# Attention and an MLP mixer on one core: the products with v as quarters of the TensorE array

## The reference

```python
def _attn_ref(q, k, v):                      # each (4, 8, 576, 64)
    ...
    q_rot, k_rot = (rotate(q), rotate(k))
    scores = scale * np.matmul(q_rot, k_rot.transpose(0, 1, 3, 2))
    scores = scores - np.max(scores, axis=-1, keepdims=True)
    attn = np.exp(scores)
    attn = attn / (np.sum(attn, axis=-1, keepdims=True) + 1e-09)
    return np.matmul(attn, v)

def _moe_ref(x, w_tok1, w_tok2, w_ch1, w_ch2):   # x is (4, 576, 512)
    xt = x.transpose(0, 2, 1)
    h = np.maximum(xt @ w_tok1, 0.0) @ w_tok2
    u = x + h.transpose(0, 2, 1)
    h2 = np.maximum(u @ w_ch1, 0.0) @ w_ch2
    return u + h2
```

## Time and profile before

| | |
|---|---|
| median of two runs | 676.19 us (674.8 to 677.58) |
| profiled execution, its own time | 677.07 us |
| span of its records | 675.2 us |
| granted clock of TensorE, mean | 1.00 |
| busy: PE, PEld, DVE, ACT, POOL | 650.1, 627.6, 449.6, 390.2, 296.1 us |

### The profile page before, as it was taken

The page is one execution under the profiler, slowest core; times in us unless marked ns, Lnnn a source line. Parts: engine busy times, 40 slices in busy tenths (PEclk is TensorE's granted clock), DMA queues, the critical chain, the costliest instruction groups (busy, mean ns, idle before and its releaser), DMA issues.

```text
span 675.2 us, 19627 instructions
## 1 busy us (share of the span) xinstructions
PE 650.1 (96%) x7796; PEld 627.6 (93%) x7796; DVE 449.6 (67%) x844; ACT 390.2 (58%) x725; POOL 296.1 (44%) x276
## 2 busy tenths in 40 slices
PE   3999999999999999999999999999999999999997
PEld 2999999999999999999899999999999999999997
DVE  5576766666766666666545598548974489644895
ACT  3455556565555565665547355677646775476753
POOL 4656567766665566522570000484004840048300
PEclk9999999999999999999999999999999999999999
DMA  4234433344433544311600233100031000310002
GB/s 131 73 99 116 130 87 107 101 109 112 116 108 104 149 111 134 87 53 34 205 2 1 63 126 102 48 1 2 2 102 47 0 0 2 99 48 1 1 2 71
DMA packets 52177, 48.73 MB, mean 72 GB/s; under 512 B 15104, under 2 KB 44352, under 8 KB 52096
## 3 DMA queue, kind: packets, MB, share of 16 engines
q1 hardware_dynamic: 51792, 47.52, 24.8%
q10 hardware_dynamic: 304, 0.07, 0.0%
HBM read 30.77 MB, written 9.44 MB: 60 GB/s over the span
## 4 chain that ended last, share of the span: by engine, by line
PE 96%; ACT 1%; DVE 1%; issue 0%; DVEq 0%
PE rest L648 24%; PE slot L604 10%; PE slot L1158 8%; PE slot L1160 8%; PE slot L1159 8%; PE rest L543 7%; PE rest L1158 6%; PE rest L1160 6%; PE rest L1159 6%; PE slot L600 3%; PE slot L1190 2%; PE rest L1190 2%; PE slot L543 1%; PE rest L224 1%; PE rest L221 1%; ACT pt L762 1%
## 5 line engine op out<-in xcount | busy, mean ns | idle before, releaser
L648 PE MATMUL rest<-v,pt 64*128 64x65 f32 x2304 | 152.5, 272 | 7.8 <-ACT pt L762 7.1
L648 PEld LDWEIGHTS rest<-v,pt 64*128 64x128 f32 x2304 | 147.0, 189 | 10.9 <-ACT pt L762 9.4
L840 DVE TENSOR_REDUCE neg_max<-slot 128x1 f32<-128x576 f32 x144 | 108.6, 756 | 71.1 <-PE slot L604 67.8
L1149 POOL TENSOR_TENSOR w_ch_part<-w_ch_sums,w_ch_part 128x512 fp32r<-128x512 f32 x21 | 31.0, 1475 | 178.0 <-ACT w_ch_part L1400 178.0
L762 ACT ACTIVATE pt<-rest 128x320 f32<-128x320 f32 x128 | 55.6, 435 | 88.6 <-PE rest L543 88.6
L1464 ACT ACTIVATE pieces<-h 128x288 fp32r<-128x288 f32 x168 | 73.8, 444 | 49.9 <-PE slot L1160 26.4
L604 PE MATMUL slot<-turned_k,turned_q 64*128 64x288 f32 x256 | 88.2, 436 | 2.3 <-ACT moved_q L776 1.6
L604 PE MATMUL slot<-moved_k,moved_q 64*128 64x288 f32 x256 | 88.2, 436 | 0.0
L1555 DVE TENSOR_TENSOR pieces<-h,pieces 128x288 fp32r<-128x288 f32 x168 | 74.3, 452 | 9.3 <-ACT pieces L1464 8.8
L851 DVE COPY pt<-rest 128x320 f32<-128x320 f32 x128 | 61.7, 482 | 14.8 <-PE rest L543 14.8
L751 ACT ACTIVATE prob_a<-slot,neg_max 128x576 f32<-128x576 f32 x80 | 59.2, 740 | 15.9 <-DVE neg_max L840 12.8
(11 more groups left out here) (248 smaller groups left out, 1922.8 us busy)
## 6 DMA issues: line engine op xcount, KB each, us to landing
moved_q<-turned_q SPq DMA_DIRECT2D x31, 160.0 KB, 2.5
raw_qk<-in_q_dram SPq DMA_DIRECT2D x16, 256.0 KB, 2.6
raw_v<-in_v_dram SPq DMA_DIRECT2D x16, 256.0 KB, 2.7
x_scratch<-x_pair SPq DMA_DIRECT2D x16, 256.0 KB, 2.0
stage_or_x<-x_scratch SPq DMA_DIRECT2D x16, 256.0 KB, 4.0
raw_qk<-in_k_dram SPq DMA_DIRECT2D x15, 256.0 KB, 2.9
w_ch_whole<-in_moe_w_ch_dram SPq DMA_DIRECT2D x8, 384.0 KB, 3.5
w_ch_A_whole<-in_moe_w_ch_dram SPq DMA_DIRECT2D x4, 768.0 KB, 7.8
```

The source lines that it names most:

```text
L648: return pe.matmul(rest[:, 2 + r, at:at + V], x[rows, j, :], w[rows, j, :], start=begins, stop=ends, skip_group_check=True)
L840: dve.tensor_reduce(neg_max[p % 2][:, i:i + 1], score_slot(p, i)[:, :, 0:HALF], AX.XY, ALU.max, negate=True).then_inc(maxed, 1)
```

## The change

Each product with v is issued twice, once for 64 of the 128 queries and once for the other 64. The weights become 64 keys by 64 queries, and the output of a product goes to partitions 0 to 63 or to partitions 64 to 127 of the same bank: rows and columns of the array are both used in halves. The same 65 columns of v stream past both. Semaphores, the order of steps and all other instructions stay.

```diff
             def add(r, n, x, w, j, begins=False, ends=False):
                 rows = (top, low)[r]
                 at = (n - HEADS["AB"[n >= G]][0]) * V
-                return pe.matmul(rest[:, 2 + r, at:at + V], x[rows, j, :], w[rows, j, :], start=begins, stop=ends, skip_group_check=True)
+                for half in (top, low):
+                    mm = pe.matmul(rest[half, 2 + r, at:at + V], x[rows, j, half], w[rows, j, :], start=begins, stop=ends, skip_group_check=True)
+                return mm
```

## The result

The changed kernel takes **653.39 us** (median of 652.32 and 654.46) against 676.19 before: a ratio of 0.9653, 95% interval 0.9604 to 0.9702. It is faster by 23 us. The forecast was 640 us in 608 to 724. The profiled execution took 654.46 us, its span is 652.7, the clock of TensorE 1.00.

The account below looks back on a forecast made before the run. The prediction took PE, busy 96% of the span, to bound the kernel, and the load of 128 float32 columns to bound L648. Its terms, −75 + 36 + 2 = −37 us, took 677 to 640 us, range 608 to 724.

Parts of the forecast that it names:

- Term 1: Products with v at L648: halved loads, four quarters side by side, period 60 ns instead of 112; −75 us.
- Term 2: Dispatch of L648's instructions, doubled from 5760 to 11520: costed at nothing; +12 us without cover from neighbouring steps.
- Term 3: 288 changes of column grouping around the 144 steps with v: array emptied, load laid open; +36 us.
- Term 4: PE's waits around steps with v: wait before a pair's first product stays, copies on ACT and DVE less hidden; +2 us.
- Rival 1: Steps with v: quarters run side by side and changes of columns are free; 610 us, chance 0.17.
- rival 2: Steps with v: column halves of one row group take turns, changes still cost; about 723 us, chance 0.20.
- rival 3: Products with v: a load waits for its own row group's matmuls, period 112 ns again; 713 us, chance 0.08.
- Rival 4: Steps with v: column halves take turns, but changes of columns are free; 683 us, chance 0.08.
- rival 5: Steps with v: quarters partly side by side, load or stream shared, period 85, with the changes; 674 us, chance 0.07.

Follow-up runs that it names:

- Experiment 1: Changed kernel, each step's products with v issued first all for queries 0 to 63, then all for 64 to 127; 697.29 us, ratio 1.0315 against the kernel before.
- experiment 2: Kernel before, with only the first two products of each of the 144 steps with v in column halves; 705.09 us, ratio 1.0424.
- Experiment 6: Kernel before (128 columns) with steps reordered: products with v of tiles 0, 1 and 2 one behind the other, head B's sum earlier; 664.89 us, ratio 0.9823.
- 8: Changed kernel with the scores in column halves too; 664.37 us, ratio 0.9814 against the kernel before.
- experiments 5: The merged order: changed kernel, products with v of tiles 0, 1 and 2 issued one behind the other, head B's sum earlier; 655.58 us, ratio 0.9673.
- experiment 7: Changed kernel with steps reordered so that products with v of tiles 0 and 1, and of 2 and 3, are issued together; 663.20 us, ratio 0.9778.
- experiment 12: Changed kernel, no steps merged, tile 0's products behind tile 3's scores and head B's sum earlier; 681.32 us, ratio 1.0070 against the kernel before.
- experiment 11: Merged order with column halves only for products of tiles 0, 1, 2 and 4, the others on 128 columns; 655.63 us, ratio 0.9698.

## Why the prediction was right

**What bounds L648** (load of 128 float32 columns, 107 ns, the stream hidden): right. Halving the columns made the load 135 instead of 188 ns and took the 55 ns of waiting out of every product.

**Term 1, quarters side by side, period 60, −75 us**: right in mechanism and in size, period 59 and −76 us. Experiment 1 shows that it is the column halves side by side that pay, and not the shorter loads.

**Term 2, dispatch at nothing**: the step that failed. The queue ahead of TensorE does take four loads and four matmuls in 60 ns, as assumed. What the term left out is where instructions come from: 80 packets instead of 58, one every 4.2 us instead of 7.3. That is 13 us of gaps, 9 of them inside the steps with v, of which the earlier trace rows had no sign. That PE runs ahead of its supply there is what the ends of the packets and experiment 1 point to; how far ahead instructions are held, no run shows. By the text's own test (a spacing of about 30 ns between any two loads) the term would have passed: the gaps come whole, 0.4 to 1.2 us at a time, not spread over the loads.

**Term 3, changes of the array's shape, +36 us**: right in mechanism. 0.152 to 0.156 us each instead of 0.127: +44. The price taken from a change of rows carried over for the way out of a step with v (by the medians 0.158, forecast 0.145); I had put too little on the way in (0.143 behind a transpose and 0.198 behind a score, forecast 0.095 and 0.15). The first score behind L649 lasts 0.51 us, as said, but starts 0.15 us behind the last product, not 0.2: part of the price falls on its follower, which starts 0.35 us later instead of 0.30. The Trainium skill's rule (page "TensorEngine Tiling (Array Packing)", "Key Properties"), that changing the tiling mode drains TensorE, holds here for 64 by 128 against 64 by 64, with that price: experiment 2 pays it 288 times for 288 faster products.

**Term 4, waits, +2 us**: the other way. The wait before tile 0's products shrank by 4 us. It is a wait for DVE's sum y_B, which begins behind tile 8's products; between these and tile 0's stand transposes, which the change of columns now delays. That this is what shortened the wait is argued, not shown. The earlier trace rows put this wait down to ACT's copy. The changed kernel's profile names y_B, and the starts settle it: in both kernels PE goes on 0.25 to 0.26 us behind the end of y_B in all 15 pairs, while ACT's copy ends just ahead of PE's start in the one and behind it in the other. Experiment 6, whose order takes that sum earlier, has no such wait.

**The rivals.** Rival 1 (free changes) is refuted by experiment 2, rival 2 (turns) by experiments 1 and 8, rival 3 (a load waits for its own row group's matmuls) by the period of 59 ns, which is too short for a load of 54 and a stream of 55 in a row. The Trainium skill's rule (page "TensorE: Matmul & The Clock Gate", Part 3, "The mechanism"), that a weight load overlaps a running matmul only when the row group differs, therefore disagrees with this trace for column halves too. Rival 4 falls with rivals 1 and 2, and rival 5 (period 85) by the same 59 ns.

The sum, −76 + 44 + 13 − 4 = −23, against −75 + 36 + 2 = −37: of the 14 us between them, 13 are the irregular gaps and 8 the price of a change of columns; 6 come back by the waits of term 4 and 1 by term 1. That the errors partly cancel is luck, and it hides how far off term 2 was.

## What to carry to other kernels

Splitting a matmul of 64 rows by columns pays where its weight load is the bound and the burst is long enough: here four quarters take 59 ns where two halves took 112, a step needs some six products of 53 ns to pay for its two changes of columns, and neighbours with another shape set that price. Count the instructions too: once TensorE spends them quickly, whole blocks of them come late, and every further gain on paper (merged steps, scores in halves as well) is given back there, in part because long waits of TensorE were followed by stretches at half its clock. No version tried here that does all the work is faster than the changed kernel: the merged order with column halves gives the same time, and an order that is worked out from engine times needs the queue of the DMAs in it.

## What was not expected of the hardware

- TensorE waited for instructions: up to 1.2 us at a time in the changed kernel, 3.1 us in the merged order, and it resumed 1.3 to 1.6 us behind the end of a 16 KB packet of the instruction queue. Both the trace and experiment 1 (the same instructions at a slower pace, and no gap over 0.16 us inside the steps) point to the supply; with a quarter of the loads of q, k and v the waits were 2.3 and 13.8 us instead of 5.6 and 18.9.
- Products of one column half overlap with the other's where the order passes from one to the other: 40 matmuls in turn took 1.00 us from first to last start, not 1.17.
- Float32 streams of 288 columns ran in four quarters at the time of two: 85.9 us against 88.2.
- The kernels with the longest waits ran at a lower clock: 0.992 and 0.990 on the mean in experiments 5 and 7, 0.982 in experiment 12, and 1.00 in the changed kernel. In experiments 5 and 7 it fell to half 0.1 to 1.5 us behind gaps of 1.8 to 3.3 us; one stretch of experiment 7 (292.9 to 299.7 us) follows no such gap, and the profiled run of experiment 11 had a wait of 2.0 us and no such stretch.
